# Moving q times d from GpSimd to VectorE in a fused attention and expert kernel, with new staging, sums and scales

## The reference

```
m_new = max(f[t] + m, i[t]);  f' = exp(f[t] + m - m_new);  i' = exp(i[t] - m_new)
C = f' * C + i' * outer(v[t], k[t]);   n = f' * n + i' * k[t]
y[t] = sigmoid(o[t]) * (C @ q[t]) / max(|n . q[t]|, 1)
```

## Time and profile before

| what | before |
|---|---|
| median of 3 runs | 419.03 us (419.0 to 421.14) |
| profiled execution, its own time | 417.85 us |
| its span, first to last instruction | 416.1 us |
| mean granted TensorE clock | 0.984 |
| TensorE busy | 386.2 us, 93% |
| VectorE busy | 283.7 us, 68% |
| ScalarE busy | 225.9 us, 54% |
| GpSimd busy | 212.2 us, 51% |

### The profile page before, as it was taken

The page is one execution under the profiler, slowest core; times in us unless marked ns, Lnnn a source line. Parts: engine busy times, 40 slices in busy tenths (PEclk is TensorE's granted clock), DMA queues, the critical chain, the costliest instruction groups (busy, mean ns, idle before and its releaser), DMA issues.

```text
span 416.1 us, 9463 instructions
## 1 busy us (share of the span) xinstructions
PE 386.2 (93%) x2741; PEld 359.5 (86%) x2742; DVE 283.7 (68%) x496; ACT 225.9 (54%) x406; POOL 212.2 (51%) x225
## 2 busy tenths in 40 slices
PE   0999996899999999999999999599999999999983
PEld 0858886789999999999999999588998999899873
DVE  8999989958656788557766676677473257874231
ACT  4647772454556545655555655546465358874230
POOL 6577978436556665342434464045264423886221
PEclk9999997899999999999999999989999999999998
DMA  7979774335255544644222254225736219741110
GB/s 198 304 286 320 231 221 147 112 83 165 76 182 172 184 134 153 189 135 166 72 71 61 66 202 143 105 64 174 277 117 260 64 40 354 262 153 36 56 36 26
DMA packets 30682, 63.43 MB, mean 152 GB/s; under 512 B 8984, under 2 KB 20763, under 8 KB 30012
## 3 DMA queue, kind: packets, MB, share of 16 engines
q1 hardware_dynamic: 28780, 57.61, 42.6%
q0 software_dynamic: 1808, 5.31, 3.8%
q10 hardware_dynamic: 64, 0.15, 0.1%
HBM read 56.40 MB, written 6.88 MB: 152 GB/s over the span
## 4 chain that ended last, share of the span: by engine, by line
PE 83%; DVE 8%; issue 2%; DMA 2%; ACT 2%; DVEq 0%; POOL 0%; SPq 0%; POOLq 0%; ACTq 0%
PE ps L1541 7%; PE ps L1543 7%; PE ps L1542 7%; PE ps L1525 5%; PE ps L1527 5%; PE ps L1526 5%; PE ps L1674 4%; PE ps L1676 4%; PE ps L1675 4%; PE ps L1631 3%; PE ps L1633 3%; PE ps L1632 3%; PE ps L1658 3%; PE ps L1532 3%; PE ps L1533 3%
## 5 line engine op out<-in xcount | busy, mean ns | idle before, releaser
L1156 DVE SCALAR_TENSOR_TENSOR gsum<-ps,soft 128x384 f32<-128x384 f32 x64 | 35.7, 557 | 51.8 <-ACT soft L897 51.5
L670 POOL TENSOR_TENSOR win_lo<-win_raw,win_hi 128x256 fp32r<-128x256 f32 x32 | 25.1, 783 | 85.6 <-DVE win_hi L1143 85.6
L889 ACT ACTIVATE soft<-ps 128x384 f32<-128x384 f32 x64 | 31.5, 492 | 68.5 <-PE ps L1533 68.4
L1541 PE MATMUL ps<-wout_hi,ghi 128*128 128x336 f32 x192 | 61.1, 318 | 1.0 <-DVE glo L1162 1.0
L1542 PE MATMUL ps<-wout_lo,ghi 128*128 128x336 f32 x192 | 60.7, 316 | 0.0
L1543 PE MATMUL ps<-wout_hi,glo 128*128 128x336 f32 x192 | 60.7, 316 | 0.0
L1525 PE MATMUL ps<-xhi,win_hi 128*128 128x384 f32 x128 | 43.6, 341 | 0.8 <-DVE gsum L1156 0.8
L1527 PE MATMUL ps<-xhi,win_lo 128*128 128x384 f32 x128 | 43.3, 338 | 0.0
L1526 PE MATMUL ps<-xlo,win_hi 128*128 128x384 f32 x128 | 43.2, 338 | 0.0
L1674 PE MATMUL ps<-split,hthi 128*128 x120 | 38.3, 319 | 1.9 <-DVE htlo L1333 1.9
L737 POOL DMA_INDIRECT out<-yout,token x15 | 17.7, 1177 | 41.3 <-DVE yout L1341 40.3
(11 more groups left out here) (214 smaller groups left out, 996.2 us busy)
## 6 DMA issues: line engine op xcount, KB each, us to landing
e1raw<-w_e SPq DMA_DIRECT2D x24, 512.0 KB
e2raw<-w_e SPq DMA_DIRECT2D x16, 640.0 KB, 5.2
win_raw<-w_in SPq DMA_DIRECT2D x32, 192.0 KB, 2.6
wout_raw<-w_out SPq DMA_DIRECT2D x32, 160.0 KB, 2.1
kq<-kq_t SPq DMA_DIRECT2D x16, 240.0 KB
wout_t<-w_out_t SPq DMA_DIRECT2D x3, 1024.0 KB, 14.1
og<-o_t SPq DMA_DIRECT2D x2, 1152.0 KB, 7.4
kr<-k_rows SPq DMA_DIRECT2D x8, 240.0 KB, 4.7
```

What stands on the lines that cost most here:

```text
L1156: dve.scalar_tensor_tensor(half(gsum, hf), ps[:, hf, 0:S // 2], 0.0, half(soft, hf), ALU.max, ALU.add).then_inc(g_done, 1)
L1541: pe.matmul(o, ghi[u][:, cols], wout_hi[u][:, :], start=False, stop=False, skip_group_check=True)
```

## The change

- `queries` moves from GpSimd to VectorE, between the scans of pair j + 2 and the weighing of pair j + 1. GpSimd's `keys` and `inputs` of the next pair wait for it. There are three v1 buffers instead of two.
- Batch 0's stage rows go from the stage tile straight to `xn`, and the n·q rows of both batches straight to `den`; `attn_rows` holds batch 1 only. The normaliser's broadcasts are awaited by tile (`rb_first`, `rb_early`, `rb_second[k]`); for batch 1 SP issues them tile by tile between the loads of dense tiles 4 and 5.
- VectorE opens tiles 0 and 2 (output gate), GpSimd tile 1. The first w_in tile is rounded on ScalarE after pair 4 and its low parts made on GpSimd in iteration 5. `first_hidden` does all products with `xhi` first.
- Batch 1's sums open themselves: the first product of each overwrites; `start_sums` and its wait for both engines' copies go there.
- In the last dense tiles the group `second(29)` is halved: one half stays ahead of `hidden(31)`, the other goes behind it.
- In routing, both scale products move from GpSimd to VectorE, with the scale chain ahead of the slot table; TensorE puts 6 of 12 scale products before the first transposes and 6 behind them. The zero products are 8 + 17 + 12 + 2 instead of 14 + 20. The second tile's transposes go into the first expert product.
- The start: zeros for two q tiles on ScalarE, `f_start` on GpSimd.

```diff
             def store_pair(j):
-                u = j % 2
+                u, b = j % 2, 2 * j // H
                 sp.wait_ge(num_done, j + 1)
                 for h in range(2):
-                    sp.dma_start(attn_rows[(2 * j + h) * D:(2 * j + h + 1) * D, :], stage[u][HALF * h:HALF * h + D, :]).then_inc(stage_stored[u], 16)
-                sp.dma_start(nq_rows[2 * j:2 * j + 2, :], stage[u][D:D + HALF + 1:HALF, :]).then_inc(stage_stored[u], 16)
+                    at = 16 * (2 * j + h - H * b)
+                    sp.dma_start(den[at:at + 16, b, :], stage[u][HALF * h + D:HALF * h + V1, :].rearrange("o (p n) -> o p n", n=NQ)).then_inc(den_stored[u], 16)
+                for h in range(2):
+                    if b == 0:
+                        for k, at, first, n in head_pieces(2 * j + h):
+                            rows = slice(HALF * h + first, HALF * h + first + n)
+                            sp.dma_start(xn[at:at + n, k, :], stage[u][rows, :]).then_inc(stage_stored[u], 16)
...
             for j in range(1, PAIRS - 1):
-                queries(j)
+                wait_queries(pool, j)
                 keys(j + 1)
                 inputs(j + 1)
+                if j == 5:
+                    split_in(0, 0)
+                    pool.wait_ge(win_split, 2)
+            wait_queries(pool, PAIRS - 1)
             output_gate(0, 1)
-            queries(PAIRS - 1)
-            output_gate(0, 2)
...
             for h in range(2):
                 scan(1, h)
+            queries(0)
             for j in range(PAIRS - 2):
                 states(j)
                 for h in range(2):
                     scan(j + 2, h)
                 if j == 4:
-                    normaliser(0, slice(0, 16 * EARLY), nq_early, 16, 0)
+                    normaliser(0, slice(0, 16 * EARLY), (1, 2), 0)
                 if j == 5:
-                    normaliser(0, slice(16 * EARLY, P), nq_loaded, 16, 1)
+                    normaliser(0, slice(16 * EARLY, P), (3,), 1)
+                queries(j + 1)
                 weigh(j + 1)
...
             states(PAIRS - 2)
-            high_in(0, 0, 16)
-            first_gate()
+            open_tile(0)
+            open_tile(2)
             normalise(0)
+            queries(PAIRS - 1)
             weigh(PAIRS - 1)
             states(PAIRS - 1)
             normalise(1)
-            low_part(0)
             normalise(2)
-            low_part(1)
-            low_part(2)
+            for k in range(KT):
+                low_part(k)
...
-            pe.wait_ge(x2_act, 3)
-            pe.wait_ge(x2_dve, 3)
-            start_sums()
-            second(FT, 0, False)
-            with pe.Fori(FT // 2, FT - 1) as i:
+            second(FT, 0, False, opens=True)
+            with pe.Fori(FT // 2, FT - 2) as i:
...
+            f = 2 * FT - 4
+            hidden(1, f + 2, 0)
+            second(f + 1, 1, False, halves=(0,))
+            hidden(1, f + 3, 1)
+            second(f + 1, 1, False, halves=(1,))
+            second(f + 2, 0, False)
             second(2 * FT - 1, 1, True)
...
+            keep_running(8, 1)
             pe.wait_ge(hot_done, B)
...
-            keep_running(14)
+            keep_running(17)
             pe.wait_ge(put_done, 1)
...
-            keep_running(20)
+            keep_running(12)
+            pe.wait_ge(put_done, 3)
+            scales(0, TT // 2)
+            keep_running(2)
...
                     last.then_inc(mm1_done, 1)
+                    if n == 0:
+                        turn_x(1, 1, xs_loaded[1], 16)
...
             turn_x(0, 0, xs_loaded[0], 16)
+            scales(TT // 2, TT)
             very_first_product()
-            scales()
             pe.wait_ge(slots_ready, 1)
-            turn_x(1, 1, xs_loaded[1], 16)
```

342 lines of the change are left out of this document (197 added, 145 removed).

## The result

The changed kernel takes 416.47 us (median of 6 runs, 415.05 to 417.56) against 420.38 for the kernel before beside it (419.0 to 423.66): ratio 0.9884, 95% interval [0.9847, 0.9922]. Faster by more than 0.5%, as forecast; the time is 5.3 us over the forecast 411.2 and 1.3 us outside the range. Two more sets of runs of the same kernel gave 0.9868 and 0.9908, and all 21 timed executions have a median of 416.05 us and lie between 412.71 and 418.54. The profiled execution took 416.05 us, span 414.3, clock 0.984.

The account below looks back on a forecast made before the run. Attention was taken as bound by TensorE, by VectorE at its end, and the dense stage by TensorE; 4.2 + 1.2 + 0.55 + 0.5 + 1.4 = 7.85 us off 417.85 gave 410.0, forecast 411.2 as median, range 408 to 415.2.

Parts of the forecast that it names:

- Part 1: Attention: q times d on VectorE makes its pair 6.41 us, under TensorE's 6.55, and ends attention earlier; 4.2 us gained.
- Two trips through DRAM go: Attention's stage rows: direct transfers end the early normaliser's wait on VectorE; counted inside the 4.2 us for attention.
- The first dense group is reordered: Start of the dense stage: one product, not two, left after the last low part; 0.3 us, inside attention's 4.2.
- GpSimd's keys and values ... lie beside weighing and state: Attention: GpSimd's 2.00 us of work fits beside VectorE's 2.20 us of weighing and state, leaving the scans free.
- VectorE becomes the bound of all of attention: Rival in attention: scans stay at 3.75 us, the pair is 6.75, giving 412.9 us; chance 0.15.
- the late broadcast: Rival at attention's end: second normaliser's broadcast lands 1.3 us late, giving 412.5 us; chance 0.12.
- Single spreads for batch two: Dense stage: tile-by-tile normaliser broadcasts cost nothing beside full TensorE; uncovered, each about 0.4 us of SP.
- Part 3: Batch change in the dense stage: self-opened sums drop six zero products and the wait; 1.2 us, bounds 1.0 and 1.2.
- Part 4: End of the dense stage: halving the last second group shortens TensorE's wait; 0.55 us, bounds 0 and 1.1.
- Part 5: Routing: moving token scales around the gather gains 0.5 us before the transposes and 1.4 us behind them.
- the clock in the first expert product: Rival in routing: half clock falls onto the first expert product, losing 1.6 us, giving 412.8; chance 0.15.
- The base: Whole kernel: runs' median taken as 1.18 us above the profiled execution, turning 410.0 into 411.2.

Follow-up runs that it names:

- e6: Changed kernel with the product of queries and d moved back to GpSimd, all else kept: 417.07 us, 0.9912 of the kernel before.
- e9: Changed kernel with first dense weights and route weights issued later, near 41 us, gates unmoved: 416.89 us, 0.9921 of the kernel before.
- e15: Changed kernel with queries 0 to 5 on GpSimd, 6 and 7 on VectorE: 414.67 us, 0.9832 of the kernel before.
- e18: Changed kernel with queries 0 to 5 on GpSimd and the late normaliser on ScalarE's queue: 415.0 us, 0.988 of the kernel before.
- e2: Changed kernel with stage rows of both batches again stored to DRAM and read back: 417.61 us, 0.991 of the kernel before.
- e1: Changed kernel with SyncE's key and value row loads issued ahead of the pair stores: 415.13 us, 0.9889 of the kernel before.
- e8: Changed kernel with first dense weights, route weights and batch 1's output gates issued behind the sixth pair's keys and values: 428.62 us, 1.0204 of the kernel before.
- e17: Changed kernel with the late normaliser's store and broadcasts issued by ScalarE instead of SyncE: 415.98 us, 0.9891 of the kernel before.
- e11: Kernel before with only the third v buffer added: 421.77 us, 1.0004 of the kernel before.
- e4: Changed kernel with batch 1's twelve normaliser broadcasts issued together ahead of dense tile 4: 416.5 us, 0.99 of the kernel before.
- e14: Changed kernel with the routing scale products back in their old place and the old zero products: 416.58 us, 0.9911 of the kernel before.
- e5: Changed kernel run again with nothing edited, as control: 414.97 us, 0.9868 of the kernel before.
- e3: Changed kernel with 17 and 4 zero products ahead of the scale products instead of 12 and 2: 414.97 us, 0.9862 of the kernel before.

## Why the prediction was wrong

Taking both kernels' profiles together, the changed kernel gains 2.7 us to A (85.9 less 83.2), loses 1.0 in batch 0 (90.3 against 91.3 on average), gains 0.8 and 0.6 in batch 1 and the last group, and 0.8 to 1.4 in routing: 3.9 to 4.5, where the sum said 7.85. The medians say 3.0 to 5.9.

- **"Part 1: 4.2 us" is the step that failed**, and with it the sentence "Eight of them: VectorE's pair becomes 5.53 + 0.88 = 6.41 us, under TensorE's 6.55. That is the step that must hold." It held (6.37) while nothing collided, and nothing came of it: with the product back on GpSimd (e6) the last low part ends at 78.81, against 79.9 in the mean with it on VectorE and the forecast 77.9, and A comes at 83.12 against 83.2. Two slips: I multiplied five pairs by VectorE's 6.41, though TensorE's 6.55 stood beside it and is the beat as soon as VectorE is the faster (6.54 and 6.58 in e9: 0.7 us over five pairs); and I did not set the product's 0.9 us against the collisions that it ends, which cost 1.1 us at most (e6) and in the kernel before mostly 0.3 to 0.5 (scans of 3.74 to 3.92 against 3.41). Over four pairs the move costs 1 us, and with queries on GpSimd the last scans even came earlier.
- **"Two trips through DRAM go ... The early normaliser no longer makes VectorE wait, inside part 1"** was given no price of its own. Of the 2.7 us to A it is the likeliest source of most: by the last low part's end the changed kernel gains 2.2 us (82.1 less 79.9), the kernels with direct stores and queries on GpSimd have it too (78.81, 79.81 and 79.83 in e6, e15 and e18), and e2, without direct stores, hasn't (81.93). That is a comparison across single profiles; e2's clock is no match for theirs, so it is not shown.
- **"The first dense group is reordered ...: 0.3"** was too small. From the last low part's end to A are 3.84 us in both profiles of the kernel before and 3.12, 3.42 and 3.12 in the changed kernel's three: 0.4 to 0.7. No run undoes the order alone.
- **"GpSimd's keys and values ... lie beside weighing and state"** failed from the fifth pair on, where the values come late. Their issue is not to blame (e1); with fewer transfers beside them the fifth pair's come in time (e8, e9). The walk also starts 0.45 us later (25.99 against 25.54): between 25.3 and 26.4 in the profiles with this code, by how long TensorE waits for a transposed weight (1.12 and 0.43 us in the first profile) and whether its clock is at half there.
- **Rival, VectorE becomes the bound of all of attention**: half true. From the sixth pair on the scans take 3.67, 3.83 and 3.92, the pairs 6.64 and more, and VectorE is busy 29.57 of 30 us while TensorE has gaps.
- **Rival, the late broadcast**: came true as to the wait, 0.6 to 2.5 us wherever stores are direct and the queries on VectorE (e8 apart, whose pairs lie apart). The prediction's reason was a store of 5.8 us from 64.6; it was issued at 66.89 and took 3.29. What I made of that (issue behind the stores) is refuted by e17 and e18.
- **"Single spreads for batch two lie beside TensorE's full dense stage: nothing"** is not borne out: batch 0 takes 90.74 to 92.26 us in the fifteen profiles with them and 89.93, 90.65 and 90.71 in the three of the kernel before and e11, and the stall is a raw weight that comes late. But with the broadcasts joined (e4) it is 90.92, so they are not shown to be the cause of the 1.0 us, only to place it.
- **Part 3, 1.2**: right at its place, 0.8 net; VectorE's choice of experts, hidden so far in the opening's gap, shows up behind it. The step that failed is "Softplus and gate work stays ahead of the next group".
- **Part 4, 0.55**: measured 0.55, with TensorE standing 0.39 us where the sum had about 0.5. That it agrees to the hundredth is luck: 0.55 was the middle of bounds of 0 and 1.1.
- **Part 5, 1.9**: the 0.5 for the gather was worked out with zero products 0.235 us apart, which is their distance at half clock, and is measured (e14 against e5) only where the old order runs at half clock; the 1.4 behind it measured 0.8, since "the wait of 0.50 goes" was wrong (283.00, 0.50 us, still there).
- **Rival, the clock in the first expert product**: it fell there in the first profile and cost 1.4 us (E to F 8.75 against 7.30). It differs between executions of one program: of the profiles with the new routing code (e3's with more zero products) ten have the clock at full from D to F and six have not. But all four with the old routing code (the kernel before twice, e11, e14) have it at half for some of that stretch, so that the change also keeps the clock up more often is a rival that these runs don't exclude.
- **The base**: "the median of the runs is 1.18 above that execution". In the runs of the kernel before beside all the later ones it was 2.5 to 3.4 (420.38 to 421.26), which by itself accounts for 1.4 to 2.2 us of the distance to the forecast time. Relative to the kernel before, the forecast was a ratio of 0.981, just outside the interval's lower end of 0.9847.

The prediction weighed a rule of the Trainium skill (SBUF — State Buffer, "SBUF: two separate sides"), that the port pair of VectorE and GpSimd is locked for a whole instruction, and priced a collision by the 0.34 us of the earlier trace rows instead where keys and values are concerned. For v the trace agrees: in e6 GpSimd's product for v, 0.99 us alone, lies wholly beside two scans (31.75, 2.44 us), and the scans take 1.12 us more (the edges of two other products touch them too); in e9, with only the end of the key product beside it, 1.01 more; in e6's last scans 0.78. The key product, in two halves, costs less even when it lies beside the scans nearly whole: from 46.09 to 49.36 in the changed kernel, it takes 3.27 us instead of 1.02 and the scans 3.67 instead of 3.38. So the small price was that of the keys and the large one that of v; which of them a move brings beside the scans decides, and why they differ was not tested.

No version is shown to beat the changed kernel. The nearest is the split of the queries, 0.9832 against 0.9908 beside it, intervals touching at 0.987; with the late normaliser moved as well it was 0.988.

Open: why broadcasts issued earlier land no earlier; what draws the place where the clock falls; where batch 0 loses its 1.0 us; how the 2.7 us of attention divide among the direct stores, the order of the first dense group and the clock; whether the last stretch differs (130.5 to 133.4 us in profiles of either kernel, no pattern found).
